# First products in the right sides' banks, state in front, inverse columns in two streams, timed GpSimd, two queues at the start

## What is computed

```python
def _attn_ref(r, k, v, w, a, b):                 # batch 4, 8 heads, 768 steps, head size 40
    state = np.zeros((B, H, D, D))
    for t in range(S):
        y[:, :, t] = np.einsum('bhd,bhde->bhe', rt, state)
        Sa = np.einsum('bhde,bhe->bhd', state, at)
        state_decay = state * wt[:, :, None, :] - np.einsum('bhd,bhe->bhde', Sa, bt)
        state = state_decay + np.einsum('bhd,bhe->bhde', vt, kt)
def reference(...):
    x = attn_out as 3072 tokens x 320
    h = x @ w_in; x = np.maximum(0.01 * h, h) @ w_out          # 320 -> 2048 -> 320
    return (sigmoid(x @ w_gate) * (x @ w_val)) @ w_out2        # 320 -> 1536 -> 320
```

## Time and profile before

| | |
|---|---|
| median of 3 runs | 1179.9 us |
| the profiled execution | 1180.9 us |
| its span | 1179.2 us |
| TensorE busy | 1038.9 us, 88% |
| VectorE busy | 598.6 us, 51% |
| ScalarE busy | 398.7 us, 34% |
| GpSimd busy | 167.6 us, 14% |
| chain that ended last | TensorE 71%, VectorE 14%, DMA 4%, SyncE's queue 4%, issue 4% |

### The profile page before, as it was taken

How to read it: one execution, slowest core, us unless ns; L and a number is a source line. 1 busy time by engine, 2 the same in 40 slices (tenths; PEclk the granted TensorE clock), 3 DMA queues, 4 the chain that set the end, 5 groups by cost and what they waited for, 6 DMA issues and landing times.

```text
span 1179.2 us, 35633 instructions
## 1 busy us (share of the span) xinstructions
PE 1038.9 (88%) x15520; PEld 888.4 (75%) x15520; DVE 598.6 (51%) x1303; ACT 398.7 (34%) x764; POOL 167.6 (14%) x221
## 2 busy tenths in 40 slices
PE   2266658788999899989999998999999999999998
PEld 2256647677777777777787877888888888888887
DVE  7787585858485748585846222434323232322322
ACT  2131344343433343334334324553322222222322
POOL 6233222222222222222200000000000000000000
PEclk9975669899999999989999999999999999999999
DMA  5656434234334333434233204330020202020000
GB/s 172 168 148 165 97 84 92 54 80 101 83 89 98 84 96 81 93 84 120 50 73 76 67 19 138 113 108 27 1 59 1 59 1 58 1 58 1 23 1 23
DMA packets 137222, 86.86 MB, mean 74 GB/s; under 512 B 99486, under 2 KB 114590, under 8 KB 137068
## 3 DMA queue, kind: packets, MB, share of 16 engines
q1 hardware_dynamic: 128764, 62.13, 21.2%
q0 software_dynamic: 8304, 22.46, 6.4%
HBM read 65.67 MB, written 18.87 MB: 72 GB/s over the span
## 4 chain that ended last, share of the span: by engine, by line
PE 71%; DVE 14%; DMA 4%; SPq 4%; issue 4%; ACT 1%; POOL 0%; DVEq 0%; ACTq 0%; POOLq 0%
PE bank L869 12%; PE bank L919 11%; PE pair L919 11%; DVE prod L1250 4%; DVE t_unit L1254 4%; PE bank L939 4%; PE bank L937 4%; PE bank L938 4%; PE bank L884 3%; PE bank L885 3%; PE bank L886 3%; PE bank L842 2%; PE bank L889 1%; PE bank L888 1%; PE bank L775 1%
## 5 line engine op out<-in xcount | busy, mean ns | idle before, releaser
L1292 DVE TENSOR_TENSOR g_lo<-g_full,g_hi 128x512 fp32r<-128x512 f32 x168 | 124.4, 740 | 213.1 <-ACT g_hi L1076 212.8
L1076 ACT CAST g_hi<-g_full 128x512 fp32r<-128x512 f32 x168 | 104.4, 621 | 134.7 <-DVE g_full L1345 131.6
L869 PE MATMUL bank<-x_hi,w_up 128*128 128x512 f32 x480 | 138.2, 420 | 6.2 <-ACT x_hi L1083 2.3
L1250 DVE TENSOR_TENSOR prod<-t_unit,p_unit 128x126 f32<-128x126 f32 (+22 forms) x372 | 110.9, 298 | 22.6 <-DMA p_unit<-p_dram 8.5
L1069 ACT ACTIVATE g_full<-bank 128x512 f32<-128x512 f32 x96 | 57.5, 599 | 187.6 <-PE bank L869 155.5
L869 PEld LDWEIGHTS bank<-x_hi,w_up 128*128 128x128 f32 x480 | 91.6, 198 | 27.6 <-issue 3.6
L1254 DVE TENSOR_TENSOR t_unit<-t_unit,prod 128x126 f32<-128x126 f32 (+22 forms) x372 | 105.6, 284 | 12.8
L884 PE MATMUL bank<-g_hi,w_dn 128*128 128x512 f32 x192 | 79.1, 412 | 15.7 <-DVE g_lo L1292 15.6
L869 PE MATMUL bank<-x_lo,w_up 128*128 128x512 f32 x288 | 86.7, 412 | 0.0
L1345 DVE TENSOR_TENSOR g_full<-pair,h_sb 128x512 f32<-128x512 f32 x36 | 24.9, 692 | 112.7 <-PE pair L919 112.0
L885 PE MATMUL bank<-g_hi,w_dn 128*128 128x512 f32 x192 | 77.0, 401 | 0.0
(11 more groups left out here) (140 smaller groups left out, 2269.1 us busy)
## 6 DMA issues: line engine op xcount, KB each, us to landing
p_unit<-p_dram SPq DMA_DIRECT2D x48, 128.0 KB, 3.0
v_tok<-in_vT SPq DMA_DIRECT2D x12, 320.0 KB, 3.1
v_sb<-in_vF SPq DMA_DIRECT2D x48, 80.0 KB
r_sb<-in_rF SPq DMA_DIRECT2D x48, 80.0 KB
x<-y_sb SPq DMA_DIRECT2D x48, 80.0 KB
x<-x_f SPq DMA_DIRECT2D x15, 256.0 KB, 3.4
out<-vru SPq DMA_DIRECT2D x24, 160.0 KB, 1.9
v_nu<-in_vN SPq DMA_DIRECT2D x22, 160.0 KB, 3.6
```

The source lines that it names most:

```text
L869: last = nc.tensor.matmul(up_bank(m)[:], lhs, rhs, start=(e == 0), stop=(e == len(products) - 1))
L1076: nc.scalar.copy(g_hi[:, m % 2], g_full[:]).then_inc(g_hi_ready, 1)
L1250: nc.vector.tensor_tensor(terms, t_unit[:, 0:m, t:t + 1].to_broadcast([P, m, rest]), p_unit[:, t, t + 1:C].unsqueeze(1).to_broadcast([P, m ...
L1292: nc.vector.tensor_tensor(g_lo[:, m % 2], g_full[:], g_hi[:, m % 2].bitcast(F32), ALU.subtract).then_inc(g_lo_ready, 1)
```

## The change

Seven edits, the diff is cut to their core (line numbers in rows of the changed order are its own):

1. `pe_first` writes into the right sides' own banks 4 and 5 at columns 320 to 479 (`first_multiplied`, `first_copied` signal it); bank 6 is no longer claimed for it.
2. TensorE's slot 1 is now `rhs_begin, sn, st, rhs_end, vrur, first`; `rhs_end` waits for ScalarE's copy of `sn`. VectorE does `st` ahead of `vrur`, ScalarE `sn` ahead of `rhs`.
3. Each column of the inverse from the third on is two multiplications and two additions, over its even and its odd rows, each stream with its own semaphores. The columns are spread over all slots; in even windows the first two stand in slot 1, in front of `st`.
4. From window 5 on GpSimd waits for the `vrur` products before it scales a and b, and for `ka` before it scales k.
5. Unit 0: stores of `p_sb` and of `t_unit` and the load of `t_sb` go half by SyncE's and half by ScalarE's queue; VectorE scales b of chunks 0 and 1; `ka` of chunk 0 comes after five columns.
6. r and v of chunks 1 to 3 are loaded at once into buffers of their own, r and v of chunk 4 in window 2.
7. SyncE's order in a window from 6 on: `load_v, store_p, load_r, store_y`, then the rest.

```diff
-        SLOT_X = [("rhs", 0), ("vrur", -1), ("st", -1), ("first", 0)]
+        SLOT_X = [("rhs", 0), ("st", -1), ("vrur", -1)]
...
                 if chunk(n + 4):
+                    if n >= 5:
+                        filled(pool, "vrur", n - 1)
                     pool_a(pool, n + 4)
-                    pool_b(pool, n + 4)
-                if chunk(n + 2):
-                    pool_k(pool, n + 2)
+                    if n >= -2:
+                        pool_b(pool, n + 4)
                 if n >= 0:
                     fetch_a(pool, n + 5)
+                if chunk(n + 2):
+                    if n >= 5:
+                        filled(pool, "ka", n + 1)
+                    pool_k(pool, n + 2)
...
+        def load_first(sp):
+            for src, to, loaded in ((vF, v_first, v_first_loaded), (rF, r_first, r_first_loaded)):
+                sp.dma_start(to[:, 0], src[0, :, 1]).then_inc(loaded, 16)
+                sp.dma_start(to[:, 1:3].rearrange("p c q t -> p (c q t)"),
+                             src[1].rearrange("p c q t -> p (c q t)")).then_inc(loaded, 16)
...
             for n in range(NT + 2):
+                if n >= 6:
+                    load_v(sp, n - 1)
+                if 1 <= n:
+                    store_p(sp, n + 3)
+                if n >= 6:
+                    load_r(sp, n - 1)
                 if n >= 2:
                     store_y(sp, n - 2)
-                    load_v(sp, n - 1)
-                    load_r(sp, n - 1)
+                if n == 2:
+                    load_v(sp, 4)
+                    load_r(sp, 4)
...
         def pe_rhs_end(pe, n):
-                wait(pe, sn_multiplied[0], n - 2)
-                wait(pe, sn_multiplied[1], n - 2)
+                wait(pe, sn_copied, n - 2)
...
         def pe_first(pe, n):
-            claim(pe, "first", n)
...
-                    last = nc.tensor.matmul(o[upper(i), q * D:(q + 1) * D], t_sb[upper(i), n % 2, q, 0:C],
-                                            rhs_sb[upper(i), q], start=True, stop=True)
+                    last = nc.tensor.matmul(pair[upper(i), q // (TQ // 2), at:at + D], t_sb[upper(i), n % 2, q, 0:C],
+                                            rhs_sb[upper(i), q], start=False, stop=True, skip_group_check=True)
...
+                        if n < 0:
+                            if n >= -2:
+                                act.wait_ge(p_low_loaded, 32)
+                            store_p_half(act, act, n + 4, 1)
...
+                        if n == -1:
+                            store_t_half(act, act, 0, 1)
+                            load_t_half(act, act, 0, 1)
...
+                for e, rows, terms in streams:
+                    wait(dve, column_ready[e], done[e])
+                    nc.vector.tensor_tensor(terms, t_unit[:, e:m:2, t:t + 1].to_broadcast([P, rows, rest]), ...
+                                            ).then_inc(column_multiplied[e], 1)
+                for e, rows, terms in streams:
+                    dve.wait_ge(column_multiplied[e], done[e] + 1)
+                    nc.vector.tensor_tensor(t_unit[:, e:m:2, t + 1:C], t_unit[:, e:m:2, t + 1:C], terms, ALU.add
+                                            ).then_inc(column_ready[e], 1)
```

More of the change, by code:

```diff
@@ L156, in rwkv_mlp_kernel @@
         diagonal_set = sem("diagonal_set")
-        column_multiplied = sem("column_multiplied")
-        column_ready = sem("column_ready")
+        column_multiplied = [sem(f"column_multiplied{i}") for i in range(2)]
+        column_ready = [sem(f"column_ready{i}") for i in range(2)]
         t_stored = sem("t_stored")
@@ L479, in load_v_nu, with store_p_half @@
                                  vN[t, i].rearrange("p c q t -> p c (q t)")).then_inc(v_nu_loaded, 16)
+        def store_p_half(engine, queue, n, h):
+            c = n % 2
+            dst = p_dram.rearrange("(h i c q) s t -> h i c s q t", h=2, i=2, c=2)
+            emptied(engine, "a", n)
+            for i in range(2):
+                rows = slice(L * i + C * h, L * i + C * h + C)
+                queue.dma_start(dst[h, i, c], p_sb[rows, c, :, C * h:C * h + C]).then_inc(p_stored[c], 16)
         def store_p(sp, n):
             if n < NT:
-                t, c = divmod(n, 2)
-                if c == 0:
-                    wait(sp, p_top_loaded, 32 * t)
-                    wait(sp, p_low_loaded, 32 * t)
-                dst = p_dram.rearrange("(h i c q) s t -> h i c s q t", h=2, i=2, c=2)
-                emptied(sp, "a", n)
+                if n % 2 == 0:
+                    wait(sp, p_top_loaded, 32 * (n // 2))
+                    wait(sp, p_low_loaded, 32 * (n // 2))
                 for h in range(2):
-                    for i in range(2):
-                        rows = slice(L * i + C * h, L * i + C * h + C)
-                        sp.dma_start(dst[h, i, c], p_sb[rows, c, :, C * h:C * h + C]).then_inc(p_stored[c], 16)
+                    store_p_half(sp, sp, n, h)
         def load_p_rows(sp, rows, signal):
@@ L1030, in act_first @@
         def act_first(act, n):
[L1031 removed]
+            act.wait_ge(first_multiplied, n + 1)
             wait(act, cross_multiplied, n)
[L1034 to L1035 removed]
+            nc.scalar.copy(u_first[:].rearrange("p (k q) d -> p k (q d)", k=2), pair_part(2)).then_inc(first_copied, 1)
         def act_cross(act, n):
@@ L1349, in vector_program @@
             dve_constants(dve)
-            for first in range(4):
-                dve_decay(dve, first)
-            for n in range(-2, NT + 6):
+            dve_decay(dve, 0)
+            dve_decay(dve, 1)
+            dve_b(dve, 0)
+            dve_b(dve, 1)
+            dve_decay(dve, 2)
+            dve_decay(dve, 3)
+            inverse_first(dve, 0)
+            inverse_columns(dve, 0, 0, 5)
+            dve_ka(dve, 0)
+            inverse_columns(dve, 0, 5, C - 1)
+            for n in range(0, NT + 6):
                 t = (n + 2) // 2
```

192 lines of the change are left out of this document (111 added, 81 removed).

## The result

The changed kernel took 1195.7 us (median of 4 runs, 1190.2 to 1204.7) beside 1178.5 us for the kernel before on the same chip: ratio 1.015, interval 1.008 to 1.023. The forecast was 1161 us, with a range of 1143 to 1178. The kernel is **slower by 17 us**, and the result lies outside the range.

The account below looks back on a forecast made before the run. The first part was taken as bound by the loop of inverse units (VectorE columns, transfers, scores), the second by TensorE and its waits. 1180.9 - 14 (first part) - 6 (second part) = 1161 us, range 1143 to 1178.

Parts of the forecast that it names:

- (b): Second part, even windows: `st` read behind two columns waiting for `p_unit` delays the `up`, mainly windows 10, 14, 18; 8.3 us added.
- The first part gives 14 us: Up to the first `up`: it comes at 155.4 instead of 169.3, 14 us less, bounds 8 and 20.
- Rival 1: Late `p_unit` stops TensorE 2 to 4 us in all six even windows; about 1177 us, chance 0.17.
- Rival 2: The second part's gaps vanish, `p_unit` early enough and ScalarE's copy hidden; 1143 us, chance 0.15.
- Rival 3: Inverse columns on VectorE: two streams only double the instructions, without overlap, 7.3 us more a unit; 1196 us, chance 0.05.
- Start to unit 0, 1.3 earlier: Start of the kernel: unit 0's columns begin 1.3 us earlier, bounds 0.7 later and 2.8 earlier.
- Unit 1 from 48.1, in 24.5 us: First part: unit 1 starts at 48.1, ends at 72.6; late w of chunk 5 might lose up to 5 us, taken as 0.
- The turn to unit 2, 13.9 us: First part, unit 1's end to unit 2's start: 13.9 us instead of 16.7, as the scores' way is hidden.
- r and v early, 1.5 of the loop: First part: early r and v carry 1.5 us of the loop; TensorE's 25.0 us of r waits may only uncover others.
- `g_lo`, 10 off: Second part: 10 of TensorE's 15.6 us waiting for `g_lo` go, with fewer columns ahead and no GpSimd beside it.
- (a): Second part, four windows with a new x block: `rhs_end` and `st` come later behind x work; 7.6 us added.
- (c): Second part: GpSimd's scaling of a beside VectorE's `vrur` costs 0; bounds 0 and 1.0 us per window.

Follow-up runs that it names:

- e1: The kernel after with the wait for `p_unit` and a unit's first two columns put back behind `st` and `vrur` in even windows; 1170.5 us, ratio 0.990.
- e9: The kernel after with only the wait for `p_unit` left ahead of `st` and `vrur`, the two columns behind them; 1186.4 us, ratio 1.008.
- e8: The kernel before with the inverse's columns in two streams and nothing else; 1172.7 us, ratio 0.995.
- e3: The kernel after with w of chunk 5 loaded ahead of the early r and v of chunks 1 to 3; 1195.8 us, ratio 1.010.
- e5: e1 with w of chunk 5 loaded ahead of the early r and v of chunks 1 to 3; 1165.1 us, ratio 0.990.
- e15: The same kernel as e5, measured again; 1164.0 us, ratio 0.987.
- e18: e5 with GpSimd's last two weight pieces of the first MLP issued only once `p_unit` of unit 2 has landed; 1160.8 us, ratio 0.984.
- e7: e1 with r and v of chunks 1 to 3 loaded as in the kernel before, not early; 1165.0 us, ratio 0.990.
- e17: The kernel before with GpSimd's two added waits (for `vrur` and `ka`), columns in one stream; 1165.2 us, ratio 0.992.
- e12: e5 with ScalarE's order sn, rhs, `x_hi`, first in new-x-block windows and VectorE's `st` ahead of `x_lo`; 1168.3 us, ratio 0.992.
- e14: e8 with GpSimd's two added waits (for `vrur` and `ka`); 1160.8 us, ratio 0.985.

## Why the prediction was wrong

Against the profiled execution of after the sum was 29 us too low: 18.5 up to the first `up` (155.4 forecast, 173.9 measured) and 10.7 behind it (-6 forecast, +4.7 measured). Two steps failed. The first turned a gain into a loss.

**The step that failed is (b), "in even windows `st` is now read behind the first two columns, which wait for `p_unit`".** Its place was right, its size was not. It was priced at 8.3 us behind the first `up`, nearly all in windows 10, 14 and 18, and at 2.1 us of VectorE's own work in the first part, 10.4 in all. Measured in the traces it is 18.5 (14.0 and 4.5, e1), and 25 to 29 in the medians. The `up` waits for `st_sum` not in three but in all seven even windows from 8 to 20, 14.8 us in all: 2.4, 2.5 and 3.0 in windows 10, 14 and 18, where 2.1, 4 and 1.6 were forecast, and 3.6, 1.2, 1.1 and 1.1 in windows 8, 12, 16 and 20, where nothing or nearly nothing was. The arrival of `p_unit` in window 14 was forecast well (442.1; 441.9 measured). What was missed is what the move does in the other windows. The wait for `p_unit` stands a slot earlier in the program, so VectorE reaches it earlier in every even window, and stands still also where `p_unit` was in time before: 6.3 us in window 8, 4.9, 3.7 and 3.5 in windows 12, 16 and 20. The two columns' own time is part of the 25 to 29 us, 4 in the traces and 10 in the medians (e9). Why the medians have more than the traces stays open.

**The other is "The first part gives 14 us".** Without the placing (e1) the first `up` comes at 169.5, beside 169.3 in the kernel before: the first part gives nothing. The terms that failed are the start, unit 1 and, above all, the turn to unit 2, below. Both signs that the prediction had named for being wrong came: unit 1 starts at 50.24, later than 50, and the first part gives less than 8 us.

**Rival 1** named the mechanism of (b) and gave it 0.17; its price of 1177 was too low by 19 us. Its sum takes off the 6 us of the second part twice (they are in the +13 already); without that it is 1185. Rival 2's terms give 1139.5 and not 1143. Rival 3 did not take place: neighbours of a column in two streams start 0.11 to 0.13 us apart and last 0.19 to 0.21, and the streams gain. That its price, 1196, is the measured time is luck. The page that the prediction names there, the Trainium skill's "VectorE: DVE Perf Modes", also says in "The DRAIN you can't avoid" that a next op that is not held starts earlier, which the prediction left out; so by that page the streams need not lose.

The other steps in their order:
- *Columns in two streams, 2.6 less a unit*: 2.5 measured in unit 0 (15.5 beside 18.0). Right; 5 us in time (e8).
- *Start to unit 0, 1.3 earlier*: 1.3 later (28.15 beside 26.86), outside the bound of 0.7. But the start scatters: in the kernels whose start is unchanged it is 26.5 to 28.1, in the versions of after 27.1 to 28.15. So no gain is shown, and a loss hardly. `p_unit` came 4.8 us after VectorE was free, 3.8 before, which gives no sign that two queues shorten the scores' way. The way from the last column to the first products took 7.6 us, 7.3 forecast.
- *Unit 1 from 48.1, in 24.5 us, of which "up to 5 us" might be lost*: from 50.2, in 29.6 us. The bound happened: 3.7 for w of chunk 5, worth 1 to 3.5 us at the end (e3, e5, e15).
- *The turn to unit 2, 13.9 us*: 22.1, the largest single miss of the first part (8.2), and none of (b): it is 23.2 in e1. GpSimd issues two weight pieces (1.4 MB) at 89.8 us, 96.5 in the kernel before, and so now ahead of `p_unit` at 94.06; e18 shows them to be 5 to 6 us of the turn. GpSimd is earlier because TensorE's order is new: in the kernel before its fetch of a (95.47) waits 3.5 us for the right sides' last products (L714, up to 94.9), which stand behind `vrur` and so behind the wait for r; in the kernel after these products are done at 86.8, before GpSimd asks for them (87.66). That is 3.5 of the 6.7 us. The rest is in front: from the unit's end to the issue of `p_unit` it is 14.2 us (79.8 to 94.06), 12.3 before, though the scores' stores now stand ahead of y, v and r.
- *r and v early, 1.5 of the loop*: no gain shown (e7). The suspicion that these 25 us of waits hide others was right.
- *`g_lo`, 10 off*: 10.3 off (15.6 to 5.3), and 12.5 us in time (e17). Right, but for one `g_lo` of 1.67 us at 213.93, beside GpSimd's scaling of k (213.83). *r, 4.0*: 2.5. *`vrur`, 5.8*: gone.
- *(a) the copy of sn, 7.6*: 5.0 in the same stretch, and none of it could be had back (e12).
- *(c) GpSimd beside `vrur`, 0*: right; see below.
- *(d) clock, -2*: none; the mean clock is 0.95 in both.

The sign followed from this. GpSimd's timing and the streams alone are worth 18 us (e14). With all the rest of the change except the placing it is 12 (e1), a difference within the uncertainty; the placing costs 29 more.

## What to carry to other kernels

A wait placed ahead of another job on an in-order engine costs what stands behind it, so list who reads each result behind it, in every stage, before putting it there, and put the state ahead of the work that nobody needs yet. The old trace tells when a transfer arrives, but not what the wait for it costs once it stands earlier in the program: price it in every window, also where it was no wait before. A long wait in a trace is not yet a cost: take it away and see what stands there instead. When an engine is freed to run ahead, look at which transfers it will now start, and next to what.

## What the runs showed of the hardware

In the kernel after GpSimd's `a` and `b` of a chunk start as VectorE reads `vrur`. Timelines of GpSimd and VectorE:
```profile
172.05 1.18 POOL L330 TENSOR_TENSOR a_sb<-a_sb,decay 128x512 f32<-128x512 f32 x1 [10.43 <-PE bank L883]
173.19 1.18 POOL L339 TENSOR_TENSOR b_sb<-b_sb,inv 128x512 f32<-128x512 f32 x1
...
172.07 1.29 DVE L1350 TENSOR_TENSOR vru<-bank,mask 128x512 f32<-128x512 f32 x2 [0.45 <-PE bank L883]
173.28 1.29 DVE L1315 TENSOR_TENSOR prod<-t_unit,p_unit 128x66 f32<-128x66 f32 x2
...
174.76 0.33 DVE L1315 TENSOR_TENSOR prod<-t_unit,p_unit 128x60 f32<-128x60 f32 x2
```
Both readings of `vrur` from PSUM run at full speed under GpSimd's multiplication (1.29 for two, as 1.28 for two at 103.58 with no GpSimd beside them). The very next pair, with both inputs in SBUF and begun while GpSimd's second multiplication ran (173.19 to 174.37), takes 1.29, where a pair of that size takes about 0.34 elsewhere (0.33 for the slightly smaller one at 174.76). This is the pair of instructions of which no row of the kernel before told anything, and it agrees with what the Trainium skill says in "SBUF — State Buffer" on the shared port pair.

Not expected was how long a small transfer (`p_unit`, four loads of 128 KB) takes beside large ones: 3.5 us from its issue to its first use with the weight pieces behind it, 8.3 with them ahead (e18, e5).

Open stays why units 1 and 2 gain so little from the streams, what makes the way from the end of unit 1 to the issue of the next `p_unit` 2 us longer, and what the three executions of after without a trace lost beyond the profiled one.
